# Channel attention and a gated feed-forward on one core: six of 34 row chunks scored with fp32r products, and the weight and token loads moved around them

## The reference

```python
qn = q / (norm(q, axis=1) + 1e-6)          # q, k, v: (2, 6016, 256)
kn = k / (norm(k, axis=1) + 1e-6)
s = kn.transpose(0, 2, 1) @ qn / tau       # (2, 256, 256)
a = exp(s - s.max(-1)); a /= a.sum(-1) + 1e-9
x = (v @ a).reshape(12032, 256)
h = x @ w_in                               # w_in: (256, 2048)
out = (h / (1 + exp(-h))) @ w_out          # w_out: (2048, 256)
```

## Time and profile before

| | |
|---|---|
| median of 3 runs | 1079.86 us (1078.62 to 1080.01) |
| the profiled execution's own time | 1079.03 us |
| its span | 1077.2 us |
| TensorE clock granted | 1.00 throughout |
| busy: TensorE, VectorE, ScalarE, GpSimd | 1072.0, 723.8, 623.0, 35.6 us |
| moved by DMA | 54.06 MB, about 400 GB/s in the first 80 us |

### The profile page before, as it was taken

One profiled execution on the slowest core, in us unless ns is written; L12 is line 12 of the kernel. 1 busy time (PEld: TensorE's weight loads), 2 busy tenths in 40 slices (PEclk: granted clock), 3 DMA queues, 4 the chain that ended last, 5 costly groups with the idle time before them and its releaser, 6 DMA issues.

```text
span 1077.2 us, 12990 instructions
## 1 busy us (share of the span) xinstructions
PE 1072.0 (100%) x4824; PEld 905.4 (84%) x4824; DVE 723.8 (67%) x943; ACT 623.0 (58%) x782; POOL 35.6 (3%) x24
## 2 busy tenths in 40 slices
PE   9999999999999999999999999999999999999998
PEld 7888888888888888888899888888888888888998
DVE  6777687567567567566688777567566566566665
ACT  6787665555565555555666565555555555555654
POOL 2460000000000000000000000000000000000000
PEclk9999999999999999999999999999999999999999
DMA  9990000200200200200200200200200200200100
GB/s 349 393 400 10 1 1 1 78 1 1 79 1 1 78 0 0 73 0 0 79 1 1 74 1 1 79 1 1 79 1 0 78 0 0 73 0 1 40 1 34
DMA packets 26140, 54.06 MB, mean 50 GB/s; under 512 B 2544, under 2 KB 7408, under 8 KB 26096
## 3 DMA queue, kind: packets, MB, share of 16 engines
q1 hardware_dynamic: 24944, 51.42, 13.1%
q10 hardware_dynamic: 1152, 2.06, 0.5%
HBM read 41.16 MB, written 12.32 MB: 50 GB/s over the span
## 4 chain that ended last, share of the span: by engine, by line
PE 99%; DMA 1%; ACTq 0%; ACT 0%; issue 0%
PE ps_o L425 16%; PE ps_o L426 16%; PE ps_o L427 16%; PE ps_h L391 14%; PE ps_h L392 14%; PE ps_h L390 14%; PE ps_o L353 7%; DMA qk<-k_dram 1%; PE ps_h L382 0%; PE ps_h L384 0%; PE ps_h L383 0%; PE ps_o L384 0%; PE ps_o L382 0%; PE ps_o L383 0%; ACTq L648 0%; PE ps_o L372 0%
## 5 line engine op out<-in xcount | busy, mean ns | idle before, releaser
L392 PE MATMUL ps_h<-b_hi,a_lo_rest 128*128 128x512 f32 (+1 forms) x504 | 194.1, 385 | 0.0
L391 PE MATMUL ps_h<-b_lo,a_hi_rest 128*128 128x512 f32 (+1 forms) x504 | 194.1, 385 | 0.0
L390 PE MATMUL ps_h<-b_hi,a_hi_rest 128*128 128x512 f32 (+1 forms) x504 | 194.0, 385 | 0.0
L840 DVE TENSOR_TENSOR h_b<-ps_h,u 128x512 f32<-128x512 f32 x96 | 66.4, 691 | 166.9 <-PE ps_h L392 166.7
L821 DVE TENSOR_TENSOR u<-ps_h,u 128x512 f32<-128x512 f32 x96 | 66.3, 691 | 142.5 <-PE ps_h L392 91.2
L627 ACT ACTIVATE h_a<-ps_h 128x512 f32<-128x512 f32 x96 | 57.5, 599 | 162.2 <-PE ps_h L392 162.2
L426 PE MATMUL ps_o<-g_lo_a,wo_hi 128*128 128x512 f32 (+1 forms) x384 | 147.9, 385 | 0.0
L425 PE MATMUL ps_o<-g_hi_b,wo_hi 128*128 128x512 f32 (+1 forms) x384 | 147.9, 385 | 0.0
L427 PE MATMUL ps_o<-g_hi_b,wo_lo 128*128 128x512 f32 (+1 forms) x384 | 147.9, 385 | 0.0
L425 PE MATMUL ps_o<-g_hi_a,wo_hi 128*128 128x512 f32 (+1 forms) x384 | 147.9, 385 | 0.0
L426 PE MATMUL ps_o<-g_lo_b,wo_hi 128*128 128x512 f32 (+1 forms) x384 | 147.8, 385 | 0.0
(11 more groups left out here) (120 smaller groups left out, 1535.7 us busy)
## 6 DMA issues: line engine op xcount, KB each, us to landing
v_raw<-v_t_dram SPq DMA_DIRECT2D x40, 256.0 KB, 3.7
out_t_dram<-v_raw SPq DMA_DIRECT2D x20, 512.0 KB, 3.0
qk<-q_dram SPq DMA_DIRECT2D x15, 384.0 KB, 11.1
qk<-k_dram SPq DMA_DIRECT2D x14, 384.0 KB, 12.0
wp_raw<-q_dram SPq DMA_DIRECT2D x8, 384.0 KB, 10.9
home<-q_dram SPq DMA_DIRECT2D x6, 384.0 KB, 11.0
home<-k_dram SPq DMA_DIRECT2D x6, 384.0 KB, 11.5
wp_raw<-k_dram SPq DMA_DIRECT2D x6, 384.0 KB, 12.9
```

What stands on the lines that cost most here:

```text
L390: nc.tensor.matmul(ps_h[:, bank, 0:n], w_hi, x_hi, start=start, stop=False, skip_group_check=True)
L391: nc.tensor.matmul(ps_h[:, bank, 0:n], w_hi, x_lo, start=False, stop=False, skip_group_check=True)
L392: return nc.tensor.matmul(ps_h[:, bank, 0:n], w_lo, x_hi, start=False, stop=stop, skip_group_check=True)
```

## The change

- Chunks 10, 13, 21, 24, 27 and 30 (`SPLIT`) are scored as three fp32r products for each fp32 one (`score_parts`). ScalarE rounds the whole chunk (`round_rows`, 1536 columns), GpSimd subtracts (`split_rows`, 1536 columns), into one of two sets of buffers, and TensorE scores the chunk three chunks later than its place (`ORDER`, `LAG`). The slot of such a chunk is free when it is split, not when it is scored.
- The tokens of step 0 and tau are loaded after chunk 11 and split earlier; the norm sums of batch 0 are one chunk later on TensorE, its row additions move from VectorE to GpSimd.
- w_in is loaded after chunks 15, 18, 21 and 24 into a buffer that becomes its `lo` half, and both rounded (a copy) and split by GpSimd, between the chunk splits.
- w_out is loaded behind the last chunk, rounded by ScalarE (two parts before the first fold copy, two in the first pair) and split by VectorE in the first pair of step 0.
- The roots of the norms stay in PSUM, VectorE's shift reads them from there, and the multiplication with 1/tau is merged into the shift. VectorE's norm chain of batch 0 is spread over the places after chunks 22 to 25, the exponentials follow after chunk 26.

```diff
+SPLIT = (10, 13, 21, 24, 27, 30)
+LAG = 3
+SETS = 2
+    ORDER = sorted(range(len(CHUNKS)), key=lambda g: (g + LAG, 1) if g in SPLIT else (g, 0))
@@ SP
-                    sp.wait_ge(chunk_scored, g - RING + 1)
+                    if g - RING in SPLIT:
+                        sp.wait_ge(rows_split, SPLIT.index(g - RING) + 1)
+                    else:
+                        sp.wait_ge(chunk_scored, PLACE[g - RING] + 1)
-                if g in (7, 10, 13, 16):
+                if g in (15, 18, 21, 24):
+                    n = (g - 15) // 3
+                    sp.dma_start(w_in_part(w_in_raw, n), w_in_parts[n // 2, n % 2]).then_inc(w_in_loaded[n], 16)
-                if g == SECOND:
+                if g == 11:
                     sp.dma_start(tau_col[:], bass.AP(tau.tensor, 0, [[0, P], [1, 1]])).then_inc(tau_loaded, 16)
                     load_v(0)
+            for n in range(PARTS):
+                sp.dma_start(wo_raw[:, n * FK // PARTS:(n + 1) * FK // PARTS, :], w_out_parts[n]).then_inc(
+                    wo_loaded[n], 16)
@@ GpSimd
+            def split_rows(n):
+                pool.wait_ge(rows_rounded, n + 1)
+                parts = [qk_parts[n % SETS][:, i].rearrange("p i r c -> p (i r c)") for i in range(2)]
+                nc.gpsimd.tensor_tensor(parts[1], qk[SPLIT[n] % RING][:, :, :, :].rearrange("p i r c -> p (i r c)"),
+                                        parts[0].bitcast(F32), ALU.subtract).then_inc(rows_split, 1)
+            def round_and_split_w_in(n):
+                pool.wait_ge(w_in_loaded[n], 16)
+                nc.gpsimd.tensor_copy(w_in_part(w_in_hi, n), w_in_part(w_in_raw, n)).then_inc(w_in_rounded, 1)
+                pool.wait_ge(w_in_rounded, n + 1)
+                nc.gpsimd.tensor_tensor(w_in_part(w_in_lo, n), w_in_part(w_in_raw, n),
+                                        w_in_part(w_in_hi, n).bitcast(F32), ALU.subtract).then_inc(w_in_split, 1)
+            split_rows(0)
             ...
+            split_rows(1)
+            split_v()
             ...
+            add_rows(0)
+            split_t12()
+            round_and_split_w_in(0)
+            split_rows(2)
+            split_t34()
+            round_and_split_w_in(1)
+            split_rows(3)
+            round_and_split_w_in(2)
+            split_rows(4)
+            round_and_split_w_in(3)
+            split_rows(5)
@@ TensorE
+            def score_parts(g):
+                ...
+                pe.wait_ge(rows_split, n + 1)
+                for r in range(ROWS):
+                    for c in range(CK):
+                        nc.tensor.matmul(out, hi[:, 1, r, d], hi[:, 0, r, :], ...)
+                        nc.tensor.matmul(out, hi[:, 1, r, d], lo[:, 0, r, :], ...)
+                        mm = nc.tensor.matmul(out, lo[:, 1, r, d], hi[:, 0, r, :], ...)
-            for g in range(len(CHUNKS)):
-                score_chunk(g)
-                if g == SECOND + 1:
+            for g in ORDER:
+                if g in SPLIT:
+                    score_parts(g)
+                else:
+                    score_chunk(g)
+                if g == SECOND + 2:
                     sum_norms(0)
@@ ScalarE
+            def round_rows(g):
+                n = SPLIT.index(g)
+                if n >= SETS:
+                    act.wait_ge(chunk_scored, PLACE[SPLIT[n - SETS]] + 1)
+                nc.scalar.activation(qk_parts[n % SETS][:, 0], qk[g % RING][:, :, :, :], ACT.Copy).then_inc(rows_rounded, 1)
             def round_wo(n):
+                act.wait_ge(chunk_scored, PLACE[SPLIT[-2]] + 1)
                 act.wait_ge(wo_loaded[n], 16)
@@ VectorE
-                link(nc.vector.tensor_scalar_add(q_scale[:], q_scale[:], 1e-6))
+                link(nc.vector.tensor_scalar_add(q_scale[:], ps_norm[:, 0:C], 1e-6))
+            def split_wo(n):
+                dve.wait_ge(wo_rounded, n + 1)
+                nc.vector.tensor_tensor(wo_part(wo_lo, n), wo_part(wo_raw, n), wo_part(wo_hi, n).bitcast(F32),
+                                        ALU.subtract).then_inc(wo_split, 1)
```

## The result

The changed kernel takes 1077.72 us (median of 22 runs, 1076.67 to 1078.29) against 1079.18 (22 runs) for the kernel before: a ratio of 0.9985, interval 0.9978 to 0.9991, 1.5 us faster. The forecast was 1.0 us. Two later comparisons, on two chips, give 0.9984 and 0.9981. The profiled execution has a span of 1075.7 us against 1077.2.

The account below looks back on a forecast made before the run. TensorE, busy 1072.0 of 1077.2 us, was taken as the bound; products 1.93, less type changes 0.2 and wait 0.7, give 1.0 us: 1079.86 - 1.0 = 1078.8 us. Range 1076.0 to 1082.5, the forecast's own 1077.9 to 1079.8.

Parts of the forecast that it names:

- rival (a): Scoring products: fp32r at 256 columns takes 109 ns, only 2.5 ns above the columns; 2.6 us gained, 1077.3 us; chance 0.24.
- part 1: Scoring on TensorE: 108 fp32r products of 126 ns replace 36 fp32 ones of 431.7 ns, gaining 1.93 us.
- The change of type: Scoring on TensorE: switching between fp32 and fp32r costs 0.04 us for both directions; five more pairs, 0.2 us.
- both extrapolations from wider products: Price of a 256-column fp32r product from 512 and 448 columns: 123 ns by a constant, 131 by a straight line.
- rival (b): Scoring products: the weight load doesn't fit behind a 107 ns stream; 3.7 to 5.7 us lost; chance 0.10.
- part 2: Loads before chunk 12: tokens put ahead land it at 29.31 us, wanted at 28.61, so TensorE waits 0.70 us.
- the tokens: Load queue before chunk 12: tau, four token loads and five rows take 2.85 us beyond the chunk's own time.
- Rival (d): Scoring stage: no gain, squares still end at 88 or chunk 12 waits 1.5 us and more; 1079.9 us; chance 0.07.
- part 3: Rounding and subtracting the six chunks: w_in copy 1.1 us; chunks 24, 27, 30 ready 1.5, 0.7 and 3.5 us early.
- Rival (c): GpSimd becomes the bound through a 2.4 us copy or slow first call; 0.3 or 2 to 4 us lost; chance 0.09.
- part 4: Norm chain and squares: with the chain spread, chunk 33's first addition is done at 82 to 84, 3 us before TensorE.
- part 5: w_out last, first pair of step 0: four VectorE subtractions, 4.8 into 4.6 us, make `h_b` 0.2 us late, costing nothing.

Follow-up runs that it names:

- r_best: Changed kernel with tokens and tau loaded after chunk 13, token sums and roundings later, exponentials after chunk 27: 1076.44 us, 0.9973 of the kernel before.
- e_fp32: Changed kernel with one fp32 product of the rounded parts in place of three fp32r products: 1080.39 us, 1.0007 of the kernel before.
- r_after: The changed kernel run again, unaltered, as yardstick beside the kernel before: 1077.99 us, 0.9984 of the kernel before.
- r_after2: The changed kernel run again, unaltered, as yardstick of a later group: 1077.46 us, 0.9981 of the kernel before.
- e_block: Changed kernel with VectorE's norm chain in one block after chunk 22 and exponentials after chunk 23: 1078.33 us, 0.9988 of the kernel before.
- e_pool: Changed kernel with GpSimd copying w_in's first two parts three times each: 1081.51 us, 1.0017 of the kernel before.
- e_dve3: Changed kernel with three extra unused reciprocals on VectorE, 5.3 us of work, after chunk 30: 1078.36 us, 0.9992 of the kernel before.
- e_spread: Kernel before with only batch 0's norm chain spread over chunks 22 to 25 and exponentials after chunk 26: 1079.50 us, ratio 0.9999.
- e_wout9: Kernel before with w_out's loads and roundings two chunks later: 1086.22 us, 1.0064 of the kernel before.

## Why the prediction was right

The gain, 1.5 us against 1.0, came the way it was worked out, by TensorE's list, but two terms were off in opposite directions. Counted from the start of the kernel before (chunk 12 wanted at 28.61), the trace has 2.53 - 1.13 = 1.40 where the forecast had 1.73 - 0.70: the list was 0.80 us better and the landing 0.4 us worse. That they partly cancel is luck. The time itself, 1077.72, is 1.1 us under the 1078.8 of the forecast, just outside its own range (from 1077.9) and nearer to the 1077.3 of rival (a); 0.68 us of that is the kernel before, whose median is 1079.18 over 22 runs and was 1079.86 over three. What tells the forecast from (a) is the traces, not the time. (One sum of the range is off: by its own terms (a) with no wait for chunk 12 is 3.3 us, not 3.5.) Term by term:

**The 108 products (part 1): size off, in favour.** 119.3 ns instead of 126. The change of type, put at 0.2 us in all, cost nothing that can be seen: chunks 32, 33 and 30 take 87.24 - 79.91 = 7.33 us, of which 5.18 are the two whole ones, so chunk 30 took 2.15 us, 18 x 119.3 ns, instead of 2.31. The part brought 2.53 us against a forecast of 1.73 (1.93 - 0.2), and 2.63 in r_best, which has no wait; e_fp32 confirms it with 2.44. The value lay below both extrapolations from wider products, 123 and 131, because neither held: from 448 to 256 columns a step falls by 0.434 ns a column, not by 0.375, and what is left on top of the columns is 12.6 ns, not the 16.0 of 448. Why is open. Rival (a), 109 ns, was refuted, and rival (b), a weight load that doesn't fit, was nearer than its chance of 0.10 said: half the columns still take 112 ns, and the product stands 7 ns above that.

**The wait for chunk 12 (part 2): place and cause right, size off, against.** 1.90 us in the trace instead of 0.70. TensorE came at 27.84 instead of 28.61, since this execution started sooner, and the landing came at 29.72 instead of 29.31. ScalarE's timeline after has the landings of chunks 11 and 12:

```profile
24.52 1.55 ACT L597 ACTIVATE ps_h<-qk 128x768 f32<-128x768 f32 x2 [0.30 <-DMA qk<-k_dram]
29.72 1.55 ACT L597 ACTIVATE ps_h<-qk 128x768 f32<-128x768 f32 x2 [3.65 <-DMA qk<-k_dram]
```

Chunk 11 landed 3.10 us sooner than before, the price of the two parts of w_out; the term that was mis-sized here is the tokens, 5.20 - 1.94 = 3.26 us instead of 2.85. By the same two landings it is 3.35, 2.81 and 3.21 us in r_after, r_after2 and e_block. What the prediction missed is that a start that differs between executions by over 1 us passes to the end in the kernel before, but an early one is swallowed by this wait in the changed one. The runs are in keeping with it: the 22 runs of before spread over 2.5 us, those of after over 1.6. Rival (d) had a wait of 1.5 us and more as a way to no gain; such a wait came, and the products more than paid for it.

**GpSimd (part 3): right.** The copy took 1.04 us, forecast 1.1; the three chunks were ready 1.4, 0.3 and 3.4 us ahead, forecast 1.5, 0.7 and 3.5. e_pool shows the first of them to be real, and what lies behind it. Rival (c) did not come. But the 0.3 us at chunk 27 last only while TensorE waits for chunk 12: in e_dve3, without that wait, TensorE waited 0.24 us for GpSimd there.

**The squares (part 4): the end right, the reason wrong.** The first addition of the last chunk was done at 83.8, forecast 82 to 84, and e_dve3 puts the lead at 3.4 us. But the step that named the spread norm chain as the cause failed in e_spread and e_block. What is left in the traces is the loads: chunk 19's squares began at 48.40 before and at 45.4 after, and the last pair at 86.26 and 81.56, so 3.0 of 4.7 us are there by chunk 19, where w_out's four parts are gone from ahead of it and two of w_in have come. That this is the cause was not tried by itself (in e_wout9 the squares were late through GpSimd's order, not through the landings), and the last 1.7 us are not taken apart. The spreading is worth at most 0.4 to 0.7 us in the changed kernel, through chunk 24's rounding.

**w_out last (part 5): right.** The four subtractions took 4.62 us, and `h_b` came 22.04 us after the first fold against 22.11 before: not late at all.

## What to carry to other kernels

Before a wide slow product is cut into several fast ones, look at what each of them costs besides its columns: here three fp32r products of 256 columns take 358 ns where an fp32 one takes 432, and at 128 columns three would still take 335. When work is put off so that the engine comes sooner for what follows it, look at the queue that feeds that next piece: moving 1 MB of tokens by two chunks and the exponentials by one was worth another 1.0 us. A chain that ends with the bound, like the squares here, must be found and given room before the bound is shortened; a change that only moves work on the engine that paces it, like the spreading, gives none.

## What the runs showed of the hardware

- A stream of fp32r products with a weight load each: 111.8 ns apart at 128 columns, 119.3 at 256, 202.7 at 448, 226.7 at 512.
- A pause of TensorE can cost more than itself. After 2.66 us of idle time (e_pool) the granted clock was 0.50 for about 3 us, at a cost of 1.2 us. e_wout9 had 4.64 us of idle time and then 0.50 as well; its first two folds took 4.42 us (93.78 to 98.20) instead of 2.80 (88.64 to 91.44 in the kernel before). Pauses of 1.73 and 2.01 us in the changed kernel left it at 1.00.
- The first chunks land at times that differ by over 1 us between executions of programs whose loads are the same (chunk 5 on TensorE from 12.28 to 13.62 us in the eight traces with the changed kernel's loads; chunk 12 landed from 29.16 to 30.19 us in them, and not in the order of the starts).
